# Queries and keys delivered features first, their low parts made on GpSimd, and a new order of work on every engine

## What is computed

```python
# 1: attention with a mask from hashed buckets; B=2, H=8, S=768, D=64
q_bits = (q @ proj > 0); k_bits = (k @ proj > 0)          # 6 bits a token
mask   = q_bucket[:, None] == k_bucket[None, :]
scores = where(mask, q @ k.T / 8, -1e9)
attn   = exp(scores - max); attn /= attn.sum() + 1e-9
x      = attn @ v                                          # 1536 tokens x 512
# 2: dense layer, 512 -> 2048 -> 512
y = (relu(x @ w_in) ** 2) @ w_out
# 3: 8 experts, each takes 192 tokens by sorted gate logits, 512 -> 1024 -> 512
```

## Time and profile before

| what | value |
|---|---|
| median of 3 runs | 862.32 us (861.07 to 863.5) |
| the profiled execution | 862.61 us, span 860.9 us |
| TensorE busy | 800.5 us (93%) |
| VectorE, ScalarE, GpSimd busy | 387.8, 376.0, 372.8 us |
| mean granted TensorE clock | 0.961 |
| attention / second layer / routing and experts | about 0 to 299 / 299 to 600 / 600 to 861 us |

### The profile page before, as it was taken

The page is one execution under the profiler, slowest core; times in us unless marked ns, Lnnn a source line. Parts: engine busy times, 40 slices in busy tenths (PEclk is TensorE's granted clock), DMA queues, the critical chain, the costliest instruction groups (busy, mean ns, idle before and its releaser), DMA issues. The chain is left out here.

```text
span 860.9 us, 14508 instructions
## 1 busy us (share of the span) xinstructions
PE 800.5 (93%) x4816; PEld 721.9 (84%) x4816; DVE 387.8 (45%) x898; ACT 376.0 (44%) x655; POOL 372.8 (43%) x302
## 2 busy tenths in 40 slices
PE   5899999999999889999999999995399999999996
PEld 3788888888887778999899999984389999999986
DVE  8557566575584235232232224224644454345400
ACT  1466766766766645554554554550011222122221
POOL 2355664665556658655564666651100111011101
PEclk8899999999999999999999999996579999999999
DMA  7265475766945000010010001001334554545451
GB/s 167 56 144 110 99 151 132 158 153 141 205 107 143 1 1 0 1 38 0 0 37 0 0 0 37 0 0 38 116 140 173 169 181 163 186 160 187 157 191 37
DMA packets 66214, 81.36 MB, mean 95 GB/s; under 512 B 41752, under 2 KB 41752, under 8 KB 65664
## 3 DMA queue, kind: packets, MB, share of 16 engines
q1 hardware_dynamic: 64128, 74.58, 31.9%
q0 software_dynamic: 2048, 6.29, 2.3%
HBM read 54.55 MB, written 6.29 MB: 71 GB/s over the span
## 5 line engine op out<-in xcount | busy, mean ns | idle before, releaser
L299 POOL TENSOR_TENSOR pt_lo<-pt,pt_hi 128x768 fp32r<-128x768 f32 x64 | 117.6, 1838 | 80.8 <-ACT pt_hi L399 68.3
L1080 PE MATMUL banks<-xt_hi,split_parts 128*128 128x384 f32 (+1 forms) x512 | 141.0, 336 | 0.0
L1091 PE MATMUL banks<-split_parts,h_hi 128*128 128x512 f32 x384 | 122.8, 401 | 3.1 <-DVE h_lo L1012 3.0
L1009 DVE TENSOR_TENSOR h<-relu 128x384 f32<-128x384 f32 x64 | 41.9, 655 | 181.4 <-ACT relu L964 181.4
L850 POOL TENSOR_TENSOR split_parts<-w_in_sb,split_parts 128x512 fp32r<-128x512 f32 x64 | 84.0, 1313 | 90.8 <-ACT split_parts L843 89.6
L392 ACT ACTIVATE pt<-banks 128x768 f32<-128x768 f32 x96 | 77.8, 810 | 54.3 <-POOL pt_lo L299 30.0
L1524 PE MATMUL banks<-x_cols,w_in_sb 128*128 128x192 f32 x512 | 96.4, 341 | 1.2 <-ACT x_cols L1304 1.1
L1080 PEld LDWEIGHTS banks<-xt_hi,split_parts 128*128 128x128 f32 x512 | 93.8, 188 | 2.5
L508 DVE TENSOR_REDUCE mx<-banks 128x1 f32<-128x768 f32 x96 | 90.1, 954 | 10.1 <-PE banks L683 6.5
L1538 PE MATMUL banks<-expert_hidden,w_out_sb 128*128 128x192 f32 x512 | 93.4, 333 | 0.0
L854 POOL TENSOR_TENSOR split_parts<-w_out_sb,split_parts 128x512 fp32r<-128x512 f32 x64 | 84.6, 1322 | 17.6 <-ACT split_parts L846 17.5
(11 more groups left out here) (181 smaller groups left out, 1363.3 us busy)
## 6 DMA issues: line engine op xcount, KB each, us to landing
w_in_sb<-in_moe_w SPq DMA_DIRECT2D x8, 2048.0 KB, 9.4
w_out_sb<-in_moe_w SPq DMA_DIRECT2D x8, 2048.0 KB, 8.2
ka<-split_parts SPq DMA_DIRECT2D x32, 192.0 KB, 3.5
qa<-split_parts SPq DMA_DIRECT2D x32, 192.0 KB, 3.6
w_in_sb<-in_moe_w_in SPq DMA_DIRECT2D x8, 512.0 KB, 6.2
w_out_sb<-in_moe_w_out SPq DMA_DIRECT2D x8, 512.0 KB, 5.9
w_out_sb<-in_k SPq DMA_DIRECT2D x16, 192.0 KB, 3.4
w_out_sb<-in_q SPq DMA_DIRECT2D x16, 192.0 KB, 4.7
```

The costliest lines, as they stand in the source:

```text
L299: pool.tensor_tensor(pt_lo[x % 2][:], pt[j % 2][:], pt_hi[x % 2][:].bitcast(fp32), ALU.subtract).then_inc(los, 1)
L1009: dve.tensor_tensor(h32[i][:], r32[i][:], r32[i][:], ALU.mult)
L1080: last = pe.matmul(PB[i][:, 0:HALF], w_[:, k, :], x_[:, xs], start=n == 0, stop=n == 3 * DT - 1)
L1091: last = pe.matmul(PB[2 + t][:], h_[:, tc], w_[:], start=start and n == 0, stop=stop and n == 2, skip_group_check=True)
```

## The change

- **Layout.** The program takes q and k with features first, `[B, NH, 64, 768]`; a load is 64 rows of 3,072 bytes, straight into the tile. The transposes `t_k`, `t_q` are gone; `k_high`, `q_high` read SBUF and wait for the load.
- **Low parts** of q and k are made on GpSimd (on VectorE for pair 0 only), in front of the pair's `low_part`s. `z_k`, `z_q` take over the transposes' waits for PSUM.
- **TensorE order.** `scores_t(2p, 0)` and `scores_t(2p, 1)` come around the last weighing of the head before; the fallbacks come directly behind; `z_k` and `z_q` are moved apart; `scores` are spread differently.
- **ScalarE order.** `expo(2p, 0)`, `k_high(p+1)`, `sums(2p-1)`, `expo(2p, 1)`, `q_high(p+1)`, `v_high(2p+1)`, `expo_high(2p, 1)`; `high(p-1)` behind `expo_high(2p, 3)`. In the last pair the first three weight splits stand behind `expo(14, 4)`.
- **GpSimd order.** `low(p-1)` behind `low_part(2p, 3)`; `divide` in two halves around `low_part(2p+1, 3)` and `(2p+1, 4)`; in the last pair the three weight splits stand in front of `divide(7, 0)`. Its drains between them are gone. The constant fills of the v tiles and the first sum over v come to GpSimd.
- **SyncE order.** After the copies for head 2p+2's `kb` and `qb` come v, q, then both heads' weights, then `part_ka(0)`, k, `part_qa(0)`. The projection is loaded from ScalarE's queue.
- **Second layer.** The transpose of the last reciprocals moves behind the second `hidden` on VectorE. The weights have two semaphores, `w_early` for the first 13 loads.

```diff
             def more_k(p):
                 if p < PAIRS:
-                    sp.wait_ge(tk, p)
+                    sp.wait_ge(kl_, p)
                     load_k(p)
...
                 if p:
+                    load_v(2 * p + 1, 1)
                     free_row(2 * p - 1, 1)
-                    load_v(2 * p + 1, 1)
-                weights(2 * p)
                 if p + 1 < PAIRS:
+                    free_row(2 * p, 0)
                     asm_kb(2 * p + 2, 0)
                     asm_qb(2 * p + 2, 0)
-                    free_row(2 * p, 0)
+                    load_v(2 * p + 2, 0)
+                more_q(p + 2)
+                weights(2 * p)
+                weights(2 * p + 1)
+                if p + 1 < PAIRS:
+                    part_ka(0)
                 more_k(p + 2)
-                if p + 1 < PAIRS:
-                    load_v(2 * p + 2, 0)
-                    part_ka(0)
-                more_q(p + 2)
-                weights(2 * p + 1)
                 if p + 1 < PAIRS:
                     part_qa(0)
```

```diff
+        def k_low(eng, p):
+            eng.wait_ge(kh_, p + 1)
+            eng.tensor_tensor(kl, k_raw, kh.bitcast(fp32), ALU.subtract).then_inc(kl_, 1)
...
             v_low_part(0, 0)
             for p in range(PAIRS):
+                if p + 1 < PAIRS:
+                    k_low(pool, p + 1)
+                    q_low(pool, p + 1)
+                low_part(2 * p, 1)
+                low_part(2 * p, 2)
+                low_part(2 * p, 3)
                 if p:
                     low(p - 1)
-                low_part(2 * p, 1)
-                low_part(2 * p, 2)
+                low_part(2 * p, 4)
                 v_low_part(2 * p + 1, 1)
-                low_part(2 * p, 3)
-                low_part(2 * p, 4)
-                divide(p)
                 low_part(2 * p + 1, 1)
                 low_part(2 * p + 1, 2)
+                if p + 1 == PAIRS:
+                    split["in_low"](pool, 0, 0, 0)
+                    split["in_low"](pool, 1, 1, 1)
+                    split["out_low"](pool, 0, 0, 0)
+                divide(p, 0)
                 low_part(2 * p + 1, 3)
                 low_part(2 * p + 1, 4)
+                divide(p, 1)
```

```diff
             for p in range(PAIRS):
-                high(p - 1)
-                sums(2 * p - 1, 1)
                 expo(2 * p, 0)
                 k_high(p + 1)
+                sums(2 * p - 1, 1)
                 expo(2 * p, 1)
                 q_high(p + 1)
+                v_high(2 * p + 1, 1)
                 expo_high(2 * p, 1)
```

```diff
             def pair(p, first, last):
+                scores_t(2 * p, 0, p, 0)
                 if not first:
-                    weigh(2 * p - 1, 1, 5)
-                    weigh_low(2 * p - 1, 1, 4, True)
-                scores_t(2 * p, 0, p, 0)
-                if not last:
-                    t_q(p + 1)
-                    t_k(p + 1)
+                    weigh_low(2 * p - 1, 1, 4)
+                    weigh(2 * p - 1, 1, 5, True)
+                scores_t(2 * p, 0, p, 1)
                 fallback(2 * p, 0, 0)
-                scores_t(2 * p, 0, p, 1)
                 fallback(2 * p, 0, 1)
                 weigh(2 * p, 0, 0)
-                scores_t(2 * p, 0, p, 2)
                 if not last:
                     z_k(p + 1)
+                scores_t(2 * p, 0, p, 2)
+                weigh_high(2 * p, 0, 1)
+                if not last:
                     z_q(p + 1)
                 scores_t(2 * p, 0, p, 3)
...
                 scores_t(2 * p + 1, 1, p, 0)
+                fallback(2 * p + 1, 1, 0)
                 if not last:
                     scores(2 * p + 2, 0, p + 1, 0, None)
-                    scores(2 * p + 2, 0, p + 1, 1, None)
-                fallback(2 * p + 1, 1, 0)
                 fallback(2 * p + 1, 1, 1)
                 scores_t(2 * p + 1, 1, p, 1)
```

More of the change, by code:

```diff
@@ L282, in _ @@
             pool.memset(turned[HIGH, :], 1.0)
+            pool.drain()
+            for i in range(2):
+                pool.memset(v_raw[i][:, :, VSL[1 - i]], 1.0)
+                pool.memset(vc[i][:, VSL[1 - i]], float(TT))
+                pool.memset(v_hi[i][:, :, VSL[1 - i]].bitcast(fp32), 1.0)
+                pool.memset(v_lo[i][:, :, VSL[1 - i]].bitcast(fp32), 0.0)
             pool.drain().then_inc(cleared, 1)
             def v_low_part(m, i):
-                pool.drain()
                 pool.wait_ge(vhs, m + 1)
@@ L299, in low_part, with divide @@
                 pool.tensor_tensor(pt_lo[x % 2][:], pt[j % 2][:], pt_hi[x % 2][:].bitcast(fp32), ALU.subtract).then_inc(los, 1)
[L301 to L307, removed]
+            def divide(g, h):
+                if h == 0:
+                    pool.wait_ge(num_, 2 * g + 1)
+                    pool.wait_ge(rec, g + 1)
+                c = slice(h * HALF, (h + 1) * HALF)
+                pool.tensor_tensor(rden[:, c], num[:, c], rden[:, c], ALU.mult).then_inc(nrm, 1)
@@ L309, in low @@
             def low(g):
                 c = slice(BLOCKS[g] * S, (BLOCKS[g] + 1) * S)
-                pool.drain()
                 pool.wait_ge(xh, g + 1)
                 pool.tensor_tensor(xt_lo[:, c], rden[:], xt_hi[:, c].bitcast(fp32), ALU.subtract).then_inc(xl, 1)
+            pool.wait_ge(v_in[0], 16)
+            parts = [pt[1][:, i * 3 * D:(i + 1) * 3 * D].rearrange("p (t d) -> p t d", d=D) for i in range(2)]
+            pool.tensor_tensor(parts[0], v_raw[0][:, 0:3, LOW], v_raw[0][:, 3:6, LOW], ALU.add)
@@ L338, in _ @@
         def _(act):
+            for i in range(2):
+                act.dma_start(proj_sb[VSL[i], :], proj).then_inc(proj_in, 16)
             act.wait_ge(made, 1)
@@ L431, in _ @@
                 expo_high(2 * p, 2)
-                v_high(2 * p + 1, 1)
                 expo(2 * p, 3)
                 expo_high(2 * p, 3)
+                high(p - 1)
                 expo(2 * p, 4)
+                if p + 1 == PAIRS:
+                    for taken in (ka_in[1], kb_in[1], qa_in[1], qb_in[1]):
+                        act.wait_ge(taken, 32 * PAIRS)
+                    act.wait_ge(split["w_early"], 16 * 13)
+                    split["in_high"](act, 0, 0)
+                    split["in_high"](act, 1, 1)
+                    split["out_high"](act, 0, 0)
+                expo_high(2 * p, 4)
                 expo(2 * p, 5)
-                expo_high(2 * p, 4)
                 row(2 * p + 1, 1)
@@ L538, in turn, with reciprocals @@
                 dve.transpose(turned[VSL[i], h * HALF:(h + 1) * HALF], O[VSL[1 - i], h, 0:HALF]).then_inc(t1, 1)
-            def invert(rows, free, done):
+            def reciprocals(rows):
                 dve.drain()
@@ L556, in pair @@
                     turn(2 * p - 1, 1, 1)
+                sum_v(2 * p + 1, 1)
                 if not last:
-                    k_low(p + 1)
-                    q_low(p + 1)
                     k_bits(p + 1).then_inc(kbits, 1)
@@ L583, in pair @@
                     v_low(2 * p + 2, 0)
-            k_low(0)
-            q_low(0)
+            k_low(dve, 0)
+            q_low(dve, 0)
             own = slice(FROW, D)
@@ L604, in _ @@
             turn(HEADS - 1, 1, 1)
[L605 removed]
+            reciprocals(HIGH)
+            dve.drain()
         @block.tensor
@@ L742, in pair @@
                 scores(2 * p + 1, 1, p, 0, None if last else p + 1)
-                weigh_high(2 * p, 0, 1)
+                weigh_low(2 * p, 0, 1)
                 scores(2 * p + 1, 1, p, 1, None if last else p + 1)
@@ L801, in _ @@
             pair(PAIRS - 1, False, True)
-            weigh(HEADS - 1, 1, 5)
-            weigh_low(HEADS - 1, 1, 4, True)
+            weigh_low(HEADS - 1, 1, 4)
+            weigh(HEADS - 1, 1, 5, True)
 def routing_constants(nc, ctx):
@@ L1585, in load_out @@
                 sp.dma_start(wo[:, part * cols:(part + 1) * cols].rearrange("p (k f) -> p k f", k=FT // 8),
-                             w_out[part * rows:(part + 1) * rows, :].rearrange("(k p) f -> p k f", p=P)).then_inc(w_ready, 16)
+                             w_out[part * rows:(part + 1) * rows, :].rearrange("(k p) f -> p k f", p=P)).then_inc(w_early if part < 5 else w_ready, 16)
             def load_gate(sp):
```

172 lines of the change are left out of this document (75 added, 97 removed).

## The result

The changed kernel takes 869.63 us (median of 10 runs, 866.04 to 873.32); before took 861.81 beside it (10 runs, 858.77 to 865.57). The ratio is 1.0085 [1.0063, 1.0107]: 0.85% slower, where I had forecast 858.9 and a range of 849 to 867. The intervals behind the ratios are 95% intervals. The profiled execution of the changed kernel took 867.50 us (span 865.8), that of before 862.61 (span 860.9).

A forecast was written before the change was run, and what follows sets the result against it. TensorE's queue was taken to bound attention. Terms -2.9 - 5.6 + 3.3 + 0.9 + 1.2 - 0.3 = -3.4 us gave 859.2 beside the profiled 862.61, or 858.9 beside the median; range 849 to 867.

The forecast's parts named there:

- start, to the first `scores_t`: Kernel start: no transposes, and v fills and sum leave VectorE, so first `scores_t` comes 2.9 us earlier (bounds 0 to 3.5).
- pair 0: First attention pair: partly at TensorE's lower level as before, waiting about what the transposes took; counted as 0.
- pairs 1, 2, 3 and 6: Four steady pairs with nothing else: 1.4 us less each, -5.6 us together.
- pairs 4 and 5, clock: Late weights delay `qa` at the next pair's start: +0.9 in pair 4, +3.3 in pair 5, +1.2 us lower clock.
- last pair and second layer: Wait before first `rows` goes, but head 15 waits for GpSimd's splits: -0.3 us, bounds -4 and +2.
- Sum 32.7 us against 34.1: 1.4 less: Walk of a steady pair's new queues: heads of 19.3 and 13.4 us, so 1.4 us less per pair.
- rival 3: Pair starts: transposes' 1.23 us only covered `sums` and `turn`, same waits show, pairs stay 34.1; 862 to 863 us; chance 0.15.
- Pairs 1 to 3 have two weight loads or none in the burst: 32.9 at most, level with the pair: Mid-pair bursts: in pairs 1 to 3 the copies let TensorE start the next pair at 32.9 us at most.
- Rival 2: Pair start: `k_high`, in front of `sums`, waits for a `ka` copy landing after 5 us; +5.8, 868 us; chance 0.18.
- The Trainium skill's rule on pieces under 512 bytes: q and k loads: larger pieces would take half the time, some 1.7 us off the burst; not counted in the forecast.

The follow-up runs named there:

- e5: Kernel before with only the layout changed: q and k features first, no transposes, all orders and SyncE's queue kept; 860.64 us, 0.9986.
- e1: Changed kernel with the even-numbered weight load, weights(2p), back early in the pair, the odd one still in the burst; 859.89 us, 0.9981 of before.
- e7: Kernel before with only SyncE's new order, both heads' weights in the mid-pair burst, q and k loads still in 256-byte pieces; 871.35 us, 1.0085.
- e10: Changed kernel with both heads' weights still late but issued behind the `qa` copy; 868.20 us, 1.0066 of before.
- e2: Changed kernel with ScalarE's sums(2p-1) in front of k_high(p+1) instead of behind it; 869.35 us, 1.0100 of before.
- e9: e8 with both weight loads early, `v_high` behind `expo_high`, and the second head's fallbacks behind the next `scores`; 852.22 us, 0.9880 of before.
- e6: Kernel before with only the transpose of the last reciprocals moved behind VectorE's second `hidden` of the second layer; 861.14 us, 0.9985.
- e11: e6 plus one line holding GpSimd's first second-layer splits until ScalarE's first high part of `h` is made; 859.32 us, 0.9967 of before.
- e8: Changed kernel with weights(2p) early, sums before k_high, GpSimd's splits last, and k_low and q_low on VectorE; 856.10 us, 0.9916 of before.

## Why the prediction was wrong

The direction was wrong, and the sum's largest term failed. Term by term, from the starts shown above against those of before, to the end of the first `rows` (316.54 us after, 309.72 before):

| term of the sum | predicted | measured |
|---|---|---|
| start, to the first `scores_t` | -2.9 | -2.7 |
| pair 0 | 0 | +1.3 |
| pairs 1, 2, 3 and 6 | -5.6 | +2.7 (138.8 against 4 x 34.0) |
| pairs 4 and 5, clock | +5.4 | +5.4 (73.5 against 68.0) |
| last pair and second layer | -0.3 | +0.1 |
| sum | -3.4 | +6.8 |

1.9 us of the 6.8 are given back by the end of the span (+4.9). They lie in the routing and the experts, which the change doesn't touch (258.9 us, 260.9 in before), and that is within what executions of one kernel differ by. The medians differ by 7.8 us; the profiled execution of the changed kernel was 2.1 us below its median, so the table explains a run of that kind and not the slower ones.

- **The start** was right. e5, whose VectorE order is that of before, starts at 25.25 us as before did, so the layout alone doesn't bring this gain; the fills and the sum that leave VectorE are the likely rest, which no run tests alone.
- **Pair 0** was taken at 0 and cost 1.3. The traces give a reason, and no run tests it. TensorE begins the pair at the lower level in both kernels: its matmuls follow each other by 0.32 us until about 30.9 us after and 29.5 before, by 0.17 from there (granted clock from 25 to 30 us 0.50 and 0.55). The pair begins 2.7 us earlier, so 8.4 us of it instead of 4.3 run at the lower level. By that the earlier start pays back about 2 us (estimate, half of 4.1), less what the missing transposes save.
- **"Sum 32.7 us against 34.1: 1.4 less" was the first step that failed**, and with it the term of -5.6. Without the waits for `qa`, pairs 1 to 6 after are 34.0, 34.6, 33.5, 33.6, 34.6 and 34.6 us, the last two with 1.3 and 1.1 us of clock in them. I had put the waits at 2.2 us and the work at 30.5. In pair 1 I read about 3.1 us of waits and slow first matmuls (1.5 us of them listed waits), so the work is nearer 30.9 by this estimate. e5 shows the mechanism by itself: the transposes stood where TensorE would have waited for the sums and low parts, and without them it waits. I had priced that as rival 3, at 0.15, though my own walk had found "a wait of 0.6 to 1.4 that the transposes covered before".
- **"Pairs 1 to 3 have two weight loads or none in the burst: 32.9 at most, level with the pair" was the second.** That number needed a burst that begins 14.9 us into the pair and drains in 18.0. In pair 2 it began at 16.7 (108.20 - 91.55) and took 19.6, so pair 3 began with a wait of 1.60 us. The late start goes with the first step: before's bursts begin 14.7 to 15.1 us into the pair, those after 15.5 to 16.9. Of that, 0.6 us is the row's DMA (`free_row`), which now stands in front of the copies, and the head in front was nowhere shorter. The burst took 1.6 us longer than the 18.0 of an equal number of bytes in before's pair 5; what that comes from stays open. Pairs 3 and 6, by the same two errors, were no shorter either.
- **The late weights in pairs 4 and 5** were right in mechanism and size: 35.4 and 38.1 us against 35.0 and 37.4. In pair 5 the closeness is partly luck: two errors cancelled, a burst 1.8 us later and 1.3 us quicker than I had it. The clock behind the waits cost about 2.4 us where I had 1.2. e1 shows that these loads are the whole net loss, e7 that they slow the old kernel as well, and e10 that issuing them behind `qa` doesn't help.
- **The last pair** was right: head 14 took 19.1 us (19.3 by the walk), head 15 19.8 (19.0), and the wait for GpSimd came where it was walked, 3.5 us.
- **Rival 2** needed late `ka` copies. There was some of it: at 94.12 `k_high` had waited 0.77 us for `ka`, and TensorE then 1.19 for the sums. e2 shows that mending the order alone buys nothing, e10 what it costs when the copy is really late.

The prediction also read the clock's digits as falling around 300 us. The earlier trace rows has no such digit; the low clock there is that of the earlier trace rows, and nothing in the sum rests on the digit.

The Trainium skill's rule on pieces under 512 bytes ("DMA: Bandwidth & Descriptors", Specifications) was set aside in the prediction, and that was too early. The q and k loads are now in large pieces (packets under 512 bytes fell from 41,752 to 17,176). Pair 5's burst moved 237 GB/s where 222 and 224 were read before, and was 1.3 us quicker than my sum without the rule; the rule's estimate was 1.7. The same queue with small pieces (e7) took 4.3 us longer in pair 5 and 5.7 in pair 4, but no longer in pairs 2 and 3. The direction agrees with the rule where the queue is fullest; the size is not shown. e5, with the large pieces and before's queue, gained nothing by them, since TensorE didn't wait for `qa` there.

## What to carry to other kernels

Work taken off the bounding engine is a gain only if what stands next in its queue is ready: before counting it, read when each input of the next three instructions is written, with the removed work gone. Bulk loads belong in the stretch of the period in which the DMA engines idle; read their share by half periods, since pair 5's mean of 0.63 held halves of 0.22 and 0.99. And when a wait's releaser is moved forward in a queue, name what it is moved past, because that is the next wait.

## What was new about the hardware

- A VectorE subtraction beside a busy GpSimd took 1.47 us instead of 0.56, a larger one 2.55 instead of 0.95, and GpSimd's own instructions stretched too (4.34 us for two low parts in e9, 3.56 in the changed kernel). The Trainium skill ("SBUF — State Buffer", Who interferes with whom) says so: a VectorE instruction with two inputs in SBUF contends with a GpSimd instruction that reads SBUF. e6 and e11 agree with it. Features first turns k and q from PSUM inputs into SBUF ones, so where their low parts stay on VectorE (e5, e8, e9) the layout brings such instructions in.
- The first single matmul behind a wait of 0.2 to 3.5 us was recorded at 0.43 to 0.45 us where the same one has 0.34 in stride, and the next one starts 0.27 to 0.29 us after it instead of 0.17 (127.76 and 57.56 in the changed kernel; the second has no wait listed).
- After waits for `qa` of 1.83 and 3.46 us the granted clock was 0.96 and 0.95 over the pair; after one of 1.60 us (pair 3) it stayed at 1.00.
